# GpSimd, not VectorE, multiplies the probabilities by the reciprocal of their sum

## The reference

```python
scores = scale * np.matmul(q, k.transpose(0, 1, 3, 2))       # q, k, v: [4, 8, 576, 64]
mask = (rel >= 0) & (rel < window)                           # rel = pos_q - pos_k, window 64
scores = np.where(mask, scores, -1000000000.0)
scores = scores - np.max(scores, axis=-1, keepdims=True)
attn = np.exp(scores)
attn = attn / (np.sum(attn, axis=-1, keepdims=True) + 1e-09)
x = attn @ v                                                  # as [2304 tokens, 512]
h = x @ moe_w_in;   x = np.maximum(0.01 * h, h) @ moe_w_out   # 512 -> 2048 -> 512
h = x @ moe2_w_in;  y = (h * np.cos(h)) @ moe2_w_out
```

## Time and profile before

| what | us |
|---|---|
| median of 3 runs | 912.01 |
| lowest and highest run | 910.81, 912.53 |
| span of the profiled execution | 910.0 |
| the runs' median less that span | 2.0 |
| TensorE (PE) busy in the span | 891.0 |
| VectorE (DVE) busy | 477.5 |
| ScalarE (ACT) busy | 393.2 |
| GpSimd (POOL) busy | 83.9 |

### The profile page before, as it was taken

The page is one execution under the profiler, slowest core; times in us unless marked ns, Lnnn a source line. Parts: engine busy times, 40 slices in busy tenths (PEclk is TensorE's granted clock), DMA queues, the critical chain, the costliest instruction groups (busy, mean ns, idle before and its releaser), DMA issues.

```text
span 910.0 us, 14462 instructions
## 1 busy us (share of the span) xinstructions
PE 891.0 (98%) x5040; PEld 846.9 (93%) x5040; DVE 477.5 (52%) x1146; ACT 393.2 (43%) x978; POOL 83.9 (9%) x68
## 2 busy tenths in 40 slices
PE   6799999999999999999999999999999999999998
PEld 5799999999999999999999889998999999999997
DVE  6755555545555554555323555545545545545543
ACT  5566444433433343434345534434433434434433
POOL 2254300000000000000256400000000000000000
PEclk9999999999999999999999999999999999999999
DMA  8455322222221222220444300100200100100100
GB/s 279 136 168 177 113 77 64 64 84 63 63 71 64 76 63 73 60 67 0 142 116 139 116 1 0 69 0 0 69 0 0 69 0 0 69 0 0 36 1 36
DMA packets 36878, 59.72 MB, mean 66 GB/s; under 512 B 3952, under 2 KB 24816, under 8 KB 36848
## 3 DMA queue, kind: packets, MB, share of 16 engines
q1 hardware_dynamic: 36848, 59.33, 21.0%
HBM read 49.87 MB, written 9.44 MB: 65 GB/s over the span
## 4 chain that ended last, share of the span: by engine, by line
PE 94%; DVE 3%; ACT 1%; issue 1%; DMA 0%; SPq 0%; ACTq 0%; DVEq 0%
PE h_ps L305 43%; PE y_ps L330 22%; PE y_ps L337 21%; PE s_ps L265 3%; PE t_ps L292 3%; PE t_ps L280 1%; DVE probs L564 1%; DVE x_raw L577 1%; DMA qk_sb<-qk 0%; DVE probs L539 0%; DVE neg_max L546 0%; DVE row_sum L552 0%; ACT w_hi L400 0%; DVE act_in L598 0%; DVE probs L596 0%
## 5 line engine op out<-in xcount | busy, mean ns | idle before, releaser
L305 PE MATMUL h_ps<-x_hi,w_hi 128*128 128x384 f32 x768 | 264.0, 344 | 1.1 <-DVE g_raw L604 0.6
L305 PE MATMUL h_ps<-x_lo,w_hi 128*128 128x384 f32 x768 | 258.3, 336 | 0.0
L305 PE MATMUL h_ps<-x_hi,w_lo 128*128 128x384 f32 x768 | 257.6, 335 | 0.0
L305 PEld LDWEIGHTS h_ps<-x_hi,w_hi 128*128 128x128 f32 x768 | 144.7, 188 | 5.9 <-DVE g_raw L604 1.0
L305 PEld LDWEIGHTS h_ps<-x_hi,w_lo 128*128 128x128 f32 x768 | 144.5, 188 | 3.7
L305 PEld LDWEIGHTS h_ps<-x_lo,w_hi 128*128 128x128 f32 x768 | 144.2, 188 | 0.3 <-DVE x_lo L583 0.3
L610 DVE TENSOR_TENSOR g_lo<-g_raw,g_hi 128x384 fp32r<-128x384 f32 x192 | 107.2, 558 | 68.4 <-ACT g_hi L448 68.4
L448 ACT ACTIVATE g_hi<-g_raw 128x384 fp32r<-128x384 f32 x192 | 100.7, 524 | 93.9 <-DVE g_raw L604 56.1
L589 DVE TENSOR_TENSOR g_raw<-h_ps,act_in 128x384 f32<-128x384 f32 x96 | 53.5, 557 | 164.4 <-ACT act_in L430 164.4
L330 PE MATMUL y_ps<-g_hi,w_hi 128*128 128x384 f32 x384 | 134.1, 349 | 0.0
L430 ACT ACTIVATE act_in<-h_ps 128x384 f32<-128x384 f32 x96 | 47.1, 490 | 194.4 <-PE h_ps L305 194.4
(11 more groups left out here) (43 smaller groups left out, 961.0 us busy)
## 6 DMA issues: line engine op xcount, KB each, us to landing
qk_sb<-qk SPq DMA_DIRECT2D x72, 224.0 KB, 2.6
v_sb<-values SPq DMA_DIRECT2D x72, 128.0 KB, 2.1
w_raw<-w_in SPq DMA_DIRECT2D x32, 256.0 KB, 2.7
w_raw<-w_out SPq DMA_DIRECT2D x32, 256.0 KB, 2.9
layer_out<-y_out SPq DMA_DIRECT2D x6, 768.0 KB, 3.8
x_raw<-layer_out SPq DMA_DIRECT2D x6, 768.0 KB, 5.2
out<-y_out SPq DMA_DIRECT2D x5, 768.0 KB, 4.0
mask_sb<-mask SPq DMA_DIRECT2D x18, 128.0 KB, 2.1
```

Source lines behind the costliest of these rows:

```text
L305: mm = pe.matmul(h_ps[j % 2][:, 0:CH], w[:, j, cols], x[:, kt, :], start=kt == 0 and a == 0, stop=kt == KT - 1 and a == 2)
```

## The change

GpSimd's code gets `normalise`, and DVE's loses it, in the start and in the chunks. GpSimd's list, so far the 64 weight halves in a row, is now written out with both kinds of work: in the start the multiplication of unit p, and from p = 5 on the half p - 5 behind it; in chunk 0 the multiplication of unit j, and two halves behind it; then the multiplications of chunks 2 to 5 in a loop; then the 32 halves of layer 2. The semaphores are the same.

```diff
--- before.py
+++ after.py
@@ -242,13 +242,37 @@
         @block.gpsimd
         def _(pool):
 
-            for u in range(4 * FT):
+            def split_half(u):
                 t, half = u // 2, u % 2
                 hi = w_hi[:, t % FT, half * DM:half * DM + DM]
                 lo = w_lo[:, t % FT, half * DM:half * DM + DM]
 
                 pool.wait_ge(w_hi_done, u + 1)
                 pool.tensor_tensor(lo, w_raw[:, u % WSTAGES, :], hi.bitcast(F32), ALU.subtract).then_inc(w_ready, 1)
+
+            def normalise(c, p):
+                r, unit = p % PRING, UNITS * c + p
+                pool.wait_ge(inv_done, unit + 1)
+                rows = probs[:, r, :].rearrange("p (a k) -> p a k", a=2)
+                inverse = bass.AP(tensor=row_inv, offset=2 * r, ap=[[2 * PRING, P], [1, 2], [0, P]])
+                pool.tensor_tensor(rows, rows, inverse, ALU.mult).then_inc(probs_done, 1)
+
+            for p in range(UNITS + 1):
+                if p < UNITS:
+                    normalise(0, p)
+                if 5 <= p < 5 + 2 * EARLY:
+                    split_half(p - 5)
+            for j in range(FT):
+                if j < UNITS:
+                    normalise(1, j)
+                if j + EARLY < FT:
+                    for half in range(2):
+                        split_half(2 * (j + EARLY) + half)
+            with nc.Fori(2, NCH, engines=(pool.engine,), hint_back_edge=True) as c:
+                for p in range(UNITS):
+                    normalise(c, p)
+            for u in range(2 * FT, 4 * FT):
+                split_half(u)
 
         @block.tensor
         def _(pe):
@@ -555,13 +579,6 @@
                 r, unit = p % PRING, UNITS * c + p
                 dve.wait_ge(sum_eps_done, unit + 1)
                 dve.reciprocal(row_inv[:, r], row_sum[:, r]).then_inc(inv_done, 1)
-
-            def normalise(c, p):
-                r, unit = p % PRING, UNITS * c + p
-                dve.wait_ge(inv_done, unit + 1)
-                rows = probs[:, r, :].rearrange("p (a k) -> p a k", a=2)
-                inverse = bass.AP(tensor=row_inv, offset=2 * r, ap=[[2 * PRING, P], [1, 2], [0, P]])
-                dve.tensor_tensor(rows, rows, inverse, ALU.mult).then_inc(probs_done, 1)
 
             def copy_o(c, p, banks):
 
@@ -658,7 +675,6 @@
                     if attends and j < UNITS:
                         add_eps(n + 1, j)
                         invert(n + 1, j)
-                        normalise(n + 1, j)
 
 
             for p in range(UNITS + 5):
@@ -673,8 +689,6 @@
                     invert(0, p - 1)
                 if 4 <= p < UNITS + 4:
                     copy_o(0, p - 4, first_banks)
-                if before:
-                    normalise(0, p - 1)
                 if p >= 7 and (p - 7) % QT == 0:
                     split_x_block(0, (p - 7) // QT)
             for j in range(LEAD):
```

## The result

| | before | after |
|---|---|---|
| median, us (9 runs each, side by side) | 912.53 | 914.34 |
| lowest and highest, us | 910.81, 913.1 | 912.56, 915.28 |
| span of the profiled execution, us | 910.0 | 912.3 |

The ratio is 1.0021, with a 95% interval of 1.0013 to 1.003. The change costs 1.8 us; 911.5 had been forecast, with 914.0 as the upper end.

A forecast was written before the change was run, and what follows sets the result against it. TensorE was taken to bound the body, with VectorE fullest in the start of under 40 us. Body 0 and start gain 0.5 us gave 912.0 - 0.5 = 911.5 us, range 909.2 to 914.0.

The forecast's parts named there:

- A change that moves VectorE's work can gain or lose in the start only: Whole kernel: TensorE bounds the body, VectorE is fullest in the start of under 40 us; body gain 0.
- the three rivals: Start hits, 909.6 us, chance 0.30; dear multiplication, 913.7, chance 0.14; later loads in the start, 912.5, chance 0.14.
- The body's multiplications cost nothing: Body: 60 multiplications leave VectorE, gain 0; at 0.68 us each the 1.76 and 1.05 us of room suffice, cost 0.
- The price on GpSimd: One 128x256 multiplication on GpSimd: 0.68 us, a fixed 0.10 and half of the other 1.17; ends 0.63 and 1.27.
- Rival (b): Multiplication takes 1.27 us on GpSimd: start +0.1, body's first units of chunks 1.6 us, time 913.7; chance 0.14.
- The tie at L552: Start, from unit 5: VectorE's small addition and GpSimd's weight half's hold both come at X + 1.37; a miss makes it wait.
- The walk: Start followed unit by unit: with misses, reciprocals of units 5 to 11 at 15.5 to 31.1; with hits, 15.5 to 29.1.
- copies on ScalarE that push the exponentials late: Start: w_hi and x_hi copies on ScalarE delay exponentials, given as the argument against the hits (909.6 us, chance 0.30).
- The start's gain: Start: last x_hi at 35.05 instead of 35.53, gain 0.5 us; with hits at 33.1, gain 2.4.
- the misses: Start: the addition waits for each weight half, 2.5 us a unit; gain 0.5 us, time 911.5, chance 0.42.
- x_lo was to be blocked twice: Start, between units 5 and 11: two blocks of VectorE's x_lo subtraction, 0.6 us for the two.
- Rival (c): Start: delayed loads and the up-projection's wait worse, as loads share the DMA; 1 us later everywhere, 912.5; chance 0.14.

The follow-up runs named there:

- e1: The changed kernel with a 128x2 memset on VectorE where each multiplication stood, so its list is as long as before: 910.35 us, ratio 0.9978.
- e12: The kernel before, nothing moved, with 104 memsets of 128x2 added on VectorE in chunk 0: 916.88 us, ratio 1.0042.
- e3: The kernel before with only the start's 12 multiplications moved to GpSimd, the body's 60 left on VectorE: 910.07 us, ratio 0.9976.
- e6: The changed kernel with VectorE memsets in place of the body's multiplications alone, its list 12 instructions shorter than before: 910.05 us, ratio 0.9981.
- e9: The changed kernel with memsets for all moved multiplications and each of the start's weight halves one unit earlier on GpSimd: 911.49 us, ratio 0.9985.
- e2: The kernel before with 92 memsets of 128x2 added on VectorE, all in chunk 5: 912.87 us, ratio 1.0007.
- e5: The changed kernel with VectorE memsets in place of the start's 12 multiplications alone, its list 24 instructions shorter than before: 914.85 us, ratio 1.0031.
- e7: The changed kernel with SP holding the next-but-one chunk's x load until layer 2 has done four down-projections: 911.38 us, ratio 0.9992.

## Why the prediction was wrong, step by step

- **"A change that moves VectorE's work can gain or lose in the start only, unless it makes TensorE wait in the body": this step failed.** It costed each engine's instructions, but not that taking 36 written instructions out of VectorE's list moves where the next block of them is loaded. TensorE was made to wait once, for 2.96 us instead of 0.55, at the entry of layer 2's loop, which none of the three rivals named. With the clock behind it the loss is 3.8 us (912.3 against e1's 908.5). e1 takes it away with no multiplication moved back, e12 makes the stall with none moved. The trace of before showed that such a wait exists, 2.67 us on ScalarE at 475.32, but nothing in it would have said that this change puts one onto VectorE at the loop, nor that it lasts 5.8 us there.
- **The body's multiplications cost nothing: right.** Between 40 and 500 us TensorE never waits for L258. In chunk 1 a reciprocal stands at 127.20 and the transposes' weights at 129.12, the room of 1.76 to 1.92 us that the earlier trace rows had. e3 leaves these 60 on VectorE, e1 and e6 have them on GpSimd: 0.9976 against 0.9978 and 0.9981.
- **The price on GpSimd: 0.68 taken, 0.61 measured.** Half of the 128x512 operation was right, without a fixed part: 1.27 less 0.61 is 0.66 for the other 256 columns. Rival (b), a dear multiplication, is out.
- **The tie at L552, now L576: missed, as the forecast had it, but in part by luck.** Timeline of after, VectorE, GpSimd and one row of ScalarE (its last read of unit 6's sums):

```profile
15.82 0.16 DVE L581 RECIPROCAL row_inv<-row_sum 128x2 f32<-128x2 f32 x1
...
16.05 0.61 POOL L258 TENSOR_TENSOR probs<-probs,row_inv 128x256 f32<-128x256 f32 x1 [0.86 <-DVE row_inv L581]
...
16.49 0.42 DVE L563 SCALAR_TENSOR_TENSOR probs<-y_ps,mask_sb 128x256 f32<-128x256 f32 x1
16.62 1.27 POOL L251 TENSOR_TENSOR w_lo<-w_raw,w_hi 128x512 fp32r<-128x512 f32 x1
...
16.71 0.19 ACT L437 ACTIVATION_READ_ACCUMULATOR probs<-probs,neg_max 128x1 f32 x1
...
16.93 0.98 DVE L576 TENSOR_SCALAR row_sum<-row_sum 128x2 f32<-128x2 f32 x1
...
29.18 1.07 DVE L576 TENSOR_SCALAR row_sum<-row_sum 128x2 f32<-128x2 f32 x1 [0.38 <-ACT probs L437]
```

  The half takes hold at about 16.74 (its row and the 0.12 us of the earlier trace rows), 0.92 us behind the reciprocal; the addition comes 1.11 behind it. The walk had 1.04 for both. So VectorE misses by 0.19 us in unit 6; in units 8, 9 and 11, by the same working (halves from 21.61, 23.95 and 28.95, additions at 21.84, 24.18 and 29.18), it misses by 0.11. Of that the cheaper multiplication gives 0.07, which the forecast did not have: at the 0.68 that it took, the miss would be about 0.04 by this estimate. In these four units the addition starts 0.03 to 0.04 us after ScalarE's last read of the sums ends (16.90 in unit 6), and at 29.18 the trace has VectorE waiting for it. The forecast blamed copies on ScalarE that push the exponentials late; only in unit 6 do they stand behind a w_hi copy without a wait, in units 8 and 9 ScalarE waited 0.99 and 0.67 us for VectorE's maximum. In units 7 and 10 it was x_lo in VectorE's own list that held the addition.
- **The start's gain: 0.5 forecast for the misses, 1.5 measured.** The pitch was nearly right: reciprocals of units 5 to 11 at 15.82, 18.16, 20.81, 23.16, 25.49, 28.16 and 30.28, 2.41 us a unit, against 15.5 to 31.1, 2.6 a unit, in the walk. The shorter multiplication gives 0.07 of the 0.19 a unit. x_lo was to be blocked twice in between; instead it slipped in between multiplication and half, and the half was the one that stretched:

```profile
18.83 0.58 DVE L600 TENSOR_TENSOR x_lo<-x_raw,x_hi 128x384 fp32r<-128x384 f32 x1
...
18.96 1.59 POOL L251 TENSOR_TENSOR w_lo<-w_raw,w_hi 128x512 fp32r<-128x512 f32 x1
...
31.72 1.06 DVE L600 TENSOR_TENSOR x_lo<-x_raw,x_hi 128x384 fp32r<-128x384 f32 x1
```

  The last of them waited 0.5 us and ended at 32.78; the walk had it blocked to 33.2, and so done at about 33.8. That is the 1.0 us by which the gain was above the forecast, and 0.8 of it is there at unit 11's reciprocal already.
- **Rival (c), later loads: there, and hidden.** TensorE's waits for queries in the start grew from 3.4 and 1.6 us to 4.2 and 2.6 (scores in either bank), and it waits 1.91 us for w_lo until 25.27, between the 25.1 and 25.7 of the walk. In e9 the wait for w_lo is gone and those for queries after 14 us are down from 1.9 to 0.4, and the start is no shorter.
- **The range** took its upper end from a dear multiplication. It missed the median by 0.3 us, and would have held 910.35, the time of the same change with the list's length kept, which the forecast of 911.5 misses by 1.2 us, for the most part the start's 1.0.

**What stays open.** Why 12 fewer instructions are harmless and 24 stall was located (the pair moves 25 us, then onto the entry), but the threshold between them wasn't. By the count that fits 12, another 12 fewer would put the pair near 501 us; it stands at 513 to 517, where 36 fewer have it too, and nothing here explains that. In e2 a single block is loaded at 515.6 us, near the entry, and nothing stalls. So that 128-instruction blocks alone explain it is not shown. The stall's 5.8 us come apart into 3.9 until the first packet starts, 2.4 of which go with the 768 KB load, and 1.9 from there to the first instruction; what these 1.9 and the other 1.5 are made of was not broken down further. The 1.4 to 1.7 us of slower clock are read from one stretch, and no run kept the gap and took the clock away.

## What to carry to other kernels

When an edit changes the number of instructions that an engine's list holds ahead of a loop, look in the trace for a wait on "issue", at loop entries above all, before believing that the edited work is to blame: a control with fillers of the same count (e1) costs one run and here turned +0.21% into -0.22%. Where such a load falls together with a large transfer, either the count or the transfer can be moved. And where two engines exclude each other, the order in the waiting engine's list decides: a small instruction that comes 0.1 to 0.2 us too late pays for what is left of the other's operation.

## What the runs showed of the hardware

- The first instruction in a loop stood 5.8 us without any semaphore to wait for, and started 1.9 us behind an 8192-byte load of instructions (1.92 or 1.93 in all five runs that stalled); with the 768 KB data load held back, 3.4 us.
- A gap of 2.96 us on TensorE was followed by 3.20 us at a clock of 0.55 (e5 and e12, gaps of 3.03 and 3.06: 6.8 us at 0.50); gaps of 1.78 (e7) and 0.55 (before) at the same place left it at 1.00.
- The mutual block of VectorE and GpSimd takes in a 2-element instruction (0.74 to 1.07 us for one of 0.17). The Trainium skill (SBUF — State Buffer, "Who interferes with whom") has the rule; that a waiting VectorE instruction gets in between two queued ones of GpSimd, and which of two then stretches, is what these rows add: 0.58 for x_lo at 18.83 and 1.59 for the half at 18.96.
